# Expert layers fed by DMA regrouping and 32x32 VectorE transposes, with the first product two slots ahead

## The reference, cut to what matters

```
N, D, E, F = 3072, 384, 8, 1024            # tokens, model, experts, inner width
for e in range(E):
    for k in range(2):
        mask = top2[:, k] == e
        h = np.maximum(x[mask] @ w1[e], 0.0)
        out[mask] += top2_w[mask, k, None] * (h @ w2[e])
# then: rms norm, silu(xn @ w_gate) * (xn @ w_val) @ w_out, width 1536
```

## Time and profile before

| what | value |
|---|---|
| median of 3 runs | 1308.37 us |
| profiled execution, its own time | 1309.53 us |
| its span in the profile | 1307.8 us |
| TensorE busy | 1244.2 us (95%) |
| VectorE busy | 858.9 us (66%) |
| ScalarE busy | 458.4 us (35%) |
| GpSimd busy | 444.2 us (34%) |

### The profile page before, as it was taken

One profiled execution on the slowest core, in us unless ns is written; L12 is line 12 of the kernel. 1 busy time (PEld: TensorE's weight loads), 2 busy tenths in 40 slices (PEclk: granted clock), 3 DMA queues, 4 the chain that ended last, 5 costly groups with the idle time before them and its releaser, 6 DMA issues.

```text
span 1307.8 us, 26515 instructions
## 1 busy us (share of the span) xinstructions
PE 1244.2 (95%) x8915; PEld 1143.2 (87%) x8916; DVE 858.9 (66%) x1941; ACT 458.4 (35%) x982; POOL 444.2 (34%) x374
## 2 busy tenths in 40 slices
PE   4999999999899999999999998699999999999998
PEld 4777878777789989899998987599999999999997
DVE  7898888876578778787877876344454444444433
ACT  3565665654232222223222222233232323233221
POOL 8467777734641606061455530311010101010000
PEclk9999999999999999999999999699999999999999
DMA  5233433245413222232314310211010101010000
GB/s 214 87 97 127 131 124 119 65 165 224 145 50 133 84 99 99 85 113 73 132 48 161 140 43 25 73 37 37 19 55 1 55 19 37 19 36 18 0 19 19
DMA packets 36175, 105.46 MB, mean 81 GB/s; under 512 B 4992, under 2 KB 20352, under 8 KB 33664
## 3 DMA queue, kind: packets, MB, share of 16 engines
q1 hardware_dynamic: 27504, 56.41, 12.9%
q0 software_dynamic: 8592, 47.98, 10.3%
HBM read 77.83 MB, written 26.54 MB: 80 GB/s over the span
## 4 chain that ended last, share of the span: by engine, by line
PE 75%; DVE 7%; POOL 6%; issue 5%; ACT 5%; DMA 2%; another core or an unknown queue 0%; DVEq 0%; SPq 0%; ACTq 0%; POOLq 0%
PE pD L1776 12%; PE pD L1885 9%; PE pA L1885 9%; PE pA L1808 9%; PE pS L1808 8%; PE pA L1899 6%; PE pA L1584 5%; PE pA L1776 5%; PE pS L1899 3%; PE pA L1790 2%; PE pX L1749 1%; POOL qk L583 1%; DVE W L1087 1%; POOL prods L599 1%; DMA stage<-w 1%
## 5 line engine op out<-in xcount | busy, mean ns | idle before, releaser
L1520 DVE TENSOR_TENSOR gs<-pD,sig 128x384 f32<-128x384 f32 x96 | 53.5, 557 | 200.3 <-ACT sig L1022 200.3
L1263 DVE STREAM_TRANSPOSE pA<-pD 32x128 f32<-32x128 f32 x416 | 138.1, 332 | 54.6 <-PE pD L1776 48.9
L751 POOL DMA_INDIRECT pair<-y_sorted,y_row x48 | 46.5, 968 | 342.9 <-DVE z L1499 272.5
L1263 DVE STREAM_TRANSPOSE pA<-pA 32x128 f32<-32x128 f32 x400 | 132.8, 332 | 43.6 <-PE pA L1776 38.0
L926 ACT ACTIVATE hidH<-pA 128x512 fp32r<-128x512 f32 x110 | 65.8, 600 | 254.5 <-DVE pA L1263 244.9
L1584 PE MATMUL pA<-W 64*128 64x128 f32 (+3 forms) x1920 | 138.0, 284 | 16.3 <-DVE W L1087 13.0
L1776 PE MATMUL pD<-we,xsH 128*128 x462 | 145.6, 396 | 0.0
L1584 PEld LDWEIGHTS pA<-W 64*128 64x128 f32 (+3 forms) x1920 | 113.8, 171 | 35.5 <-DVE W L1087 18.7
L1022 ACT ACTIVATE sig<-pD 128x384 f32<-128x384 f32 x96 | 47.1, 491 | 211.2 <-PE pA L1885 211.1
L1808 PE MATMUL pA<-we,hidH 128*128 (+1 forms) x464 | 120.9, 342 | 0.0
L1087 DVE TENSOR_TENSOR W<-W,prods 128x512 f32<-128x512 f32 (+1 forms) x120 | 102.7, 862 | 20.9 <-PE pA L1584 17.1
(11 more groups left out here) (262 smaller groups left out, 2875.2 us busy)
## 6 DMA issues: line engine op xcount, KB each, us to landing
stage<-w POOLq DMA_DIRECT2D x14, 1536.0 KB
qk<-qk_t SPq DMA_DIRECT2D x24, 512.0 KB, 3.8
xs<-x_sorted SPq DMA_DIRECT2D x55, 192.0 KB, 2.4
y_sorted<-yo SPq DMA_DIRECT2D x55, 192.0 KB, 1.9
fT<-f_t SPq DMA_DIRECT2D x12, 512.0 KB, 5.7
vN<-v_n SPq DMA_DIRECT2D x24, 256.0 KB, 2.6
out<-fin SPq DMA_DIRECT2D x8, 576.0 KB, 2.8
stage<-w SPq DMA_DIRECT2D x2, 1536.0 KB
```

The source lines that it names most:

```text
L751: pool.indirect_dma_start(out=pair[:, j, k], out_offset=None, in_=y_sorted[:, :], in_offset=bass.IndirectOffsetOnAxis(ap=y_row[:, t * TS + ...
L1263: ins = dve.transpose(by_32[1][32 * q:32 * (q + 1), :, i], by_32[0][32 * i:32 * (i + 1), :, q])
L1520: dve.tensor_tensor(gs[:], pD[:, f % 2 * 512:f % 2 * 512 + TT], sig[f % 2][:], ALU.mult).then_inc(s_u, 1)
```

## The change

It does five things.

1. x, from slot 5 on: instead of one load of 128 rows, four loads (`in_quarters`). Load q fills partitions 32q to 32q+31: partition 32q+t gets, for each of four groups j, columns 96q to 96q+95 of row 32j+t. One VectorE instruction on 128x384 then turns all 32x32 blocks (`turn_x`), and the result in `pX` is the turned x, its columns taken with a step of 3; the rows of w1 are ordered to suit.
2. The middle activation, slots 5 to 53: relu of both halves, then a store of `hid` (128 x 4 KB) to `hid_rows` in device memory, then four loads by quarters back into `hidP`, then two VectorE instructions on 128x512 (`turn_hidden`). Slots 0 to 4 and 54 are turned by TensorE, eight transposes each.
3. TensorE's slot t is now `hidden(t+2)`, `output(t)`.
4. SyncE's slot t is now `load_hidden(t+1)`, `store_rows(t-1)`, `load_rows(t+4)`, `store_hidden(t+2)`.
5. GpSimd waits for the first product before it overwrites w1 and for the second before w2. In the last layer `combine` and the mean squares are spread, one group of 128 tokens for each of three steps f.

```diff
+def in_quarters(rows):
+    return rows.rearrange("(j t) (q c) -> q t j c", t=QP, q=Q)      # QP = 32, Q = 4
...
 # SyncE
             def load_rows(t):
                 row = sp.value_load(slot_i[0:1, 1, bass.ds(t.times(1), 1)], min_val=0, max_val=E * REGION - P)
-                sp.dma_start(xs[t.c % 4][:], x_sorted[bass.ds(row, P), :]).then_inc(s_xs[t.c % 4], 16)
+                of = x_sorted[bass.ds(row, P), :]
+                if x_by_pe(t): ...
+                for q in range(Q):
+                    sp.dma_start(xs[t.c % 4][QP * q:QP * (q + 1)].rearrange("p (j c) -> p j c", j=Q),
+                                 in_quarters(of)[q]).then_inc(s_xp[t.c % 4], 16)
+            def store_hidden(t):
+                wait_alone(sp, s_relu, t.times(2, 2))
+                if t.c >= FIRST_P + 2:
+                    wait_alone(sp, s_hp, (t - FIRST_P).times(16 * Q, -16 * Q))
+                sp.dma_start(hid_rows[t.par], hid[:]).then_inc(s_hs, 16)
+            def load_hidden(t):
+                wait_alone(sp, s_hs, (t - FIRST_P).times(16, 16))
+                wait_alone(sp, s_ht, t.times(1))
+                for q in range(Q):
+                    sp.dma_start(hidP[QP * q:QP * (q + 1)].rearrange("p (j c) -> p j c", j=Q),
+                                 in_quarters(hid_rows[t.par])[q]).then_inc(s_hp, 16)
             def slot(t):
-                if (t + 4).before(SLOTS):
-                    wait_alone(sp, s_tx, t.times(1, 1))
-                    load_rows(t + 4)
-                store_rows(t)
+                if (t + 1).before(SLOTS) and not hidden_by_pe(t + 1):
+                    load_hidden(t + 1)
+                store_rows(t - 1)
+                if (t + 4).before(SLOTS):
+                    wait_alone(sp, s_tx, t.times(1, 1))
+                    load_rows(t + 4)
+                if (t + 2).before(SLOTS) and not hidden_by_pe(t + 2):
+                    store_hidden(t + 2)
 # ScalarE, rectify: both halves, hid is free once its store has landed
+                elif t.c > FIRST_P:
+                    act.wait_ge(s_hs, (t - FIRST_P).times(16))
 # VectorE
+            def turn_x(t):
+                dve.wait_ge(s_xp[t.c % 4], (t - FIRST_P).over(4, 16 * Q, 16 * Q))
+                dve.wait_ge(s_xl, t.times(1))
+                dve.transpose(pX[:, 0:DM].rearrange("p (k j t) -> p k j t", k=KC, j=Q),
+                              xs[t.c % 4].rearrange("p (j f k) -> p k j f", j=Q, k=KC)).then_inc(s_tx, 1)
+            def turn_hidden(t, h):
+                if h == 0:
+                    dve.wait_ge(s_hp, (t - FIRST_P).times(16 * Q, 16 * Q))
+                dve.wait_ge(s_hl, t.times(2, h - 1))
+                k = FC // 2
+                dve.transpose(pA[0][:, h].rearrange("p (k j t) -> p k j t", k=k, j=Q),
+                              hidP.rearrange("p (j k f) -> p k j f", j=Q, k=FC)[:, h * k:(h + 1) * k]
+                              ).then_inc(s_ht if h else s_th, 1)
 # TensorE
             def slot(t):
-                if (t + 1).before(SLOTS):
-                    hidden(t + 1)
                 if (t + 2).before(SLOTS):
-                    turn_rows(t + 2)
-                if (t + 1).before(SLOTS):
+                    hidden(t + 2)
+                if (t + 1).before(SLOTS) and hidden_by_pe(t + 1):
                     turn_hidden(t + 1)
                 output(t)
```

More of the change, by code:

```diff
@@ L362, in program @@
         s_xs = [sem(f"s_xs{i}") for i in range(4)]
+        s_xp = [sem(f"s_xp{i}") for i in range(4)]
+        s_hs = sem("s_hs")
+        s_hp = sem("s_hp")
         s_ys = [sem(f"s_ys{i}") for i in range(2)]
@@ L420, in slots @@
         def slots(eng, body):
-            for n in range(EARLY, EARLY + 3):
+            for n in range(EARLY + 1, EARLY + 3):
                 body(Tile(n))
@@ L544, in _, with slot @@
             load_rows(Tile(4))
[L545 to L549, removed]
+            for n in (1, 2, 3):
+                wait_alone(sp, s_tx, n + 1)
+                load_rows(Tile(n + 4))
+                store_rows(Tile(n))
+            wait_alone(sp, s_tx, 5)
+            load_rows(Tile(8))
+            store_hidden(Tile(5))
+            load_hidden(Tile(5))
+            store_hidden(Tile(6))
+            def slot(t):
+                if (t + 1).before(SLOTS) and not hidden_by_pe(t + 1):
[6 more added lines that the diff above has]
+                    store_hidden(t + 2)
+            slots(sp, slot)
+            store_rows(Tile(SLOTS - 1))
             def store_tile(t):
@@ L974, in _ @@
             rectify(Tile(4))
+            high_x(Tile(6))
             for h in range(2):
                 high_h(Tile(4), h)
+            rectify(Tile(5))
+            high_x(Tile(7))
+            take_rows(Tile(4))
+            rectify(Tile(6))
+            for h in range(2):
+                high_h(Tile(5), h)
             def slot(t):
-                if (t + 1).before(SLOTS):
-                    rectify(t + 1)
+                if (t + 3).before(SLOTS):
+                    high_x(t + 3)
                 if (t + 2).before(SLOTS):
-                    high_x(t + 2)
+                    rectify(t + 2)
                 if (t + 1).before(SLOTS):
@@ L1038, in wide @@
                 for f in range(F2C):
-                    if f == 4 and (t + 1).before(NT2):
-                        mean_square(t + 1)
+                    if NEXT_SUM < f <= NEXT_SUM + TS and (t + 1).before(NT2):
+                        square_of(t + 1, f - NEXT_SUM - 1)
+                    if f == NEXT_SUM + TS + 1 and (t + 1).before(NT2):
+                        root(t + 1)
                     if NEXT_Z <= f < NEXT_Z + KC and (t + 1).before(NT2):
@@ L1454, in _ @@
             low_x(Tile(4))
+            turn_x(Tile(5))
             low_x(Tile(5))
[L1456 removed]
+            turn_x(Tile(6))
+            low_x(Tile(6))
             for h in range(2):
                 low_h(Tile(4), h)
+            turn_x(Tile(7))
+            low_x(Tile(7))
+            for h in range(2):
+                turn_hidden(Tile(5), h)
+            for h in range(2):
+                low_h(Tile(5), h)
             def slot(t):
+                if (t + 3).before(SLOTS):
+                    turn_x(t + 3)
+                    low_x(t + 3)
                 if (t + 1).before(SLOTS):
[L1462 to L1466 removed]
+                    if not hidden_by_pe(t + 1):
+                        for h in range(2):
+                            turn_hidden(t + 1, h)
                     for h in range(2):
@@ L1546, in wide @@
                 for f in range(F2C):
-                    if f == 3 and more:
-                        combine(t + 1)
-                    if f == 6 and more:
+                    if NEXT_SUM <= f < NEXT_SUM + TS and more:
+                        combine(t + 1, f - NEXT_SUM)
+                    if f == NEXT_Z - 1 and more:
                         norm(t + 1)
```

152 lines of the change are left out of this document (75 added, 77 removed).

## The result

The changed kernel takes 1318.77 us (median of 4 runs, 1315.43 to 1320.64), the kernel before, run beside it, 1308.51 us (4 runs, 1305.78 to 1309.28). The ratio is 1.0084, with a 95% interval of 1.0065 to 1.0102: slower by 0.8%, and the interval lies clear of the 0.3% bound. Forecast were 1322 us. The profiled execution took 1315.43 us, its span is 1314.0 us.

The account below looks back on a forecast made before the run. SyncE's queue was to bound the expert layer at 8.7 us a slot; with 43 us of delays the layer ends 18.0 later. 1309.5 + 18.0 - 4.0 = 1323.5 us profiled, given as 1322; range 1284 to 1375.

Parts of the forecast that it names:

- The bound moved to SyncE's queue: Expert layer: SyncE's ordered queue, ten DMAs a slot, sets the time at 8.7 us against TensorE's 8.38.
- The cycle, 8.7 us: SyncE's queue, one hidden store to the next: 2.6 + 1.9 + 0.7 + 2.9 + 0.5 + 0.1 us.
- The sign was forecast to turn at 8.4 us: SyncE's cycle in the expert layer: at 8.4 us, 47 cycles give 14 us and slower turns to faster.
- the queue keeps pace: Rival for the expert layer: cycle at most 8.38 us, TensorE sets it, only weight loads cost; 1299 us, chance 0.2.
- the lookahead's 6.9 us: Hidden's path through memory takes 9.9 of 16.8 us; the 6.9 us of slack is spent once.
- The delays, 43 us: Expert layer: hidden stores landing late beside weight loads, eight after the first, add 5 x 6.5 + 3 x 3.5 us.
- The five behind the experts' pairs: Hidden stores beside pairs of 1.5 MB weight loads: each landing put off by 6.5 us.
- The turn by packets: DMA queues taking turns per packet would make delays 15 us lower; rejected for the rows, rival at 1308, chance 0.1.
- The three behind the last layer's matrices: Hidden stores beside the 2.25 MB weight loads: each landing put off by some 3.5 us.
- The sum: Expert layer: first store at 363.5, cycles 408.9, delays 43, last slots; end at 832.4 us, 18.0 later.
- The last layer gave back: Last layer: spreading combine removes the eight waits behind it at f=3, 4.0 us less.
- the dear-quarters rival: SyncE's quarter loads cost up to 0.61 us each to issue, cycle 9.5 to 10.5; 1360 to 1407 us, chance 0.15.

Follow-up runs that it names:

- read_twice: The changed kernel with the row table read twice for each row load on SyncE's queue; 1353.23 us, ratio 1.0353 to the kernel before.
- rows_between: The changed kernel with SyncE's row loads, one slot further ahead, between hidden's store and its loads; 1277.40 us, ratio 0.9781 to the kernel before.
- small_weights: The changed kernel with the twelve weight loads for experts 2 to 7 moving only 16 columns each; 1282.31 us, ratio 0.9803 to the kernel before.
- the pieces experiment in after's order: The changed kernel, SyncE's order kept, with each weight load split by columns into four DMAs; 1312.95 us, ratio 1.0082 to the kernel before.
- x_only: The changed kernel with the middle activation turned by TensorE, only x through DMA quarters and VectorE; 1297.45 us, ratio 0.9954 to the kernel before.
- wide_only: The kernel before with only the last layer's combine and mean squares spread over three steps f; 1301.86 us, ratio 0.9956.

## Why the prediction was right, step by step

**The bound moved to SyncE's queue.** Right, and shown twice: 0.6 us more of register work made the cycle 0.6 us longer (read_twice), and the same ten DMAs a slot in another order gave back 41 us (rows_between). The first load comes 0.19 us behind the landing, as forecast, and the row loads stand directly before the store.

**The cycle, 8.7 us.** The mechanism right, the sum 0.35 us high: the undisturbed cycles are mostly 8.25 to 8.5, mean 8.35. The terms, forecast and measured: landing 2.6 and 2.64; wait before the loads 0.2 and 0.19; four loads 1.9 and 1.74; y store with its register work 0.7 and 0.63; y store's end to the row loads' end 2.9 and 2.76; wait before the store 0.3 and 0.30. These make 8.26, without the branch, which was put at 0.1. The landing was taken a little too low, the others at what they are or too high, the four loads and the row loads most (back to back the rows gave 0.49 us between starts, not 0.48). Over 47 cycles 16.4 us. The sign was forecast to turn at 8.4 us, and the cycle is below that: with 8.35 in it and all else as forecast, the sum gives a kernel 2 us faster than before. That it is slower nevertheless is due to the delays (7.3 us over the forecast) and the last slots (3.2 over), below. The first rival, "the queue keeps pace", had its condition met, a cycle of at most 8.38, and yet did not come true. Its first premise failed since TensorE's slot, too, is shorter than forecast (4.18 + 4.12 = 8.30), so that the queue stays just the longer of the two. Its second, that the lookahead's 6.9 us come off the delays, needs a queue that runs ahead; this one began at the landing of store(5) with nothing ahead and gained nothing on TensorE afterwards.

**The delays, 43 us.** Eight landings beside weight loads of 10.0, 7.9, 8.4, 9.6, 9.2, 8.0, 9.4 and 7.9 us made their cycles longer by 7.5, 5.8, 6.2, 6.9, 6.6, 5.2, 6.8 and 5.3 us: 50. The five behind the experts' pairs were forecast at 32.5 and measured 33.0; that this fits so well is partly luck, since the price came from a row load that meets the weight load in another way (see "The turn by packets"). The three behind the last layer's matrices were mis-sized: 17.3 us instead of 10.5. Their price had been read from a single row load and y store, issued at other moments of the load, and a store of 512 KB behind eight more DMAs does not meet it the same way. small_weights confirms the size of the five: 33.1 us less at the layer's end without them.

**The sum.** store_hidden(6) came at 363.1 (forecast 363.5), store_hidden(53) at 805.6 (815.4): 16.4 less from the cycle, 7.3 more from the delays, 0.4 from the start, which makes 9.5 of the 9.8. From there to the end of the layer took 20.2 us instead of 17.0, since TensorE, which last waited at 768.8 and then took 5.86 us for a product at the lower clock, was itself the later one from there on. The end, 825.8, is 6.6 under the forecast. The last layer gave back 4.9 instead of 4.0. So the forecast of 1322 us, 3 us from the 1318.8 measured, owes its closeness in part to errors that cancel: 16.4 us too much for the cycles against 7.3 and 3.2 too little for the delays and the last slots. The bound and the eight delays were right; that the sign came out right as well was a matter of a few us.

**The turn by packets.** Here the reason in the text was wrong, though the number it kept was right for the five pairs. The rows were said not to agree with the rule of the Trainium skill ("DMA: Bandwidth & Descriptors", Queues, rings and completion order), that each DMA engine takes turns between its queues packet by packet. They do take such turns. What the estimate of 3.4 us left out shows in before's queues between 453.4 and 456.7 us, where the weight load runs alone although a y store had been issued at 452.75 and a row load at 454.10:

```profile
q0 software_dynamic: 87, 1.07, 86.5%
```

Only from 456.8 us does the other queue appear beside it. So the y store waits 4 us, then has its eight packets per engine in turn with the weights' at 0.5 us each, nearly 4, and an end of 1.4 (the rest of the 1.9 us that it takes alone; an estimate): about 9, as in the earlier trace rows. The row load comes behind it in the same queue. In after the hidden store comes later in the load, and behind its own queue's backlog. The queues' tables of 582 to 589 us, beside the weight load, and of 590 to 594, when it is through, read

```profile
q0 software_dynamic: 218, 2.48, 92.2%
q1 hardware_dynamic: 219, 0.21, 9.7%
```

```profile
q1 hardware_dynamic: 1002, 1.03, 79.9%
q0 software_dynamic: 9, 0.00, 0.2%
```

219 packets against 218: turns one for one, so here the trace agrees with the rule. But in those 7 us the queue gets 14 packets per engine, and ahead of the store of 584.46 stand the pieces of three hidden loads (the first had landed at 581.2), a y store and four row loads: 24 + 8 + 32 per engine, less some six already served. So the store is served when the weight load is over, at about 590, and lands 4 us later. That also fits the pieces experiment in after's order: with packets of half the size the queue gets some more turns, but the load as a whole ends no sooner. The argument is from counts; no run changed the backlog alone. Nor does any run tell why the other queue is not served at the start of a load. In after it depends on the load: beside that of 512.92 the other queue gets next to nothing for 3.5 us, beside that of 578.90 it is served from the start.

**What needed no mending.** VectorE's transposes at 0.70 us (taken 0.75) lie in TensorE's shadow, with VectorE at 3.85 of 8.30 us. The quarters are issued in 0.32 to 0.43 us, no dearer than whole rows, so the dear-quarters rival fell with its first rows. GpSimd's edit costs nothing that a wait of TensorE's shows. TensorE's waits for ScalarE come with the late landings.

**What stays open.** The first product takes 4.12 or 4.13 us in the kernels built on after whose chain is shown here, also with transposes beside it (x_only), and 4.21 in before. That alone makes 4 us over the layer. In before the two halves are released by waits of their own and in after by others; none of the runs separates that.

## What to carry to other kernels

An engine that issues in order and must wait for the landing of its own store should have other issues to make in that time: the same ten DMAs cost 0.8% in one order and gained 2.2% in the other (the last layer's 0.4% is in both). A lookahead covers a delay only once; what counts is by how much the part that runs ahead (here the queue) is shorter than the one that sets the pace (here TensorE), since that alone refills it, and small delays beat one large only when it does. When work moves from a busy engine to DMAs, price the queue that issues them, instruction by instruction, and the landings beside the largest transfers of the kernel, before the engine's own saving.

## What the runs showed of the hardware that was not expected

- VectorE's transpose in 32x32 blocks takes 701 ns on 128x384 read with a stride and 705 ns on 128x512: the smaller one is no cheaper. On 32x128 it took 332 ns.
- A DMA by quarters with three dimensions on both sides costs SyncE 0.32 us (x) or 0.32 to 0.43 us (hidden) to issue, against 0.34 for a whole-row load.
- Beside each of the five pairs of weight loads in before, the y store issued 0.5 to 0.6 us ahead of the load's first packet and the row load behind it are not served for its first 3 to 3.5 us. In after this is so beside some loads and not beside others.
- Seven of TensorE's waits in after (1.9 to 6.6 us) are followed by a second product of 5.9 to 6.6 us instead of 4.18, with 0.50 granted right behind one of them (594.5 to 597.5 us). The layer ends 58 us later than the 767.9 that its products alone would give (771.7, less 0.08 for each of 48 first products): 41.9 are the waits, some 12 these seven products, and the rest is smaller.
- The length of the wait alone does not decide it. Before's last product of the layer came after a wait of 2.0 us and took 6.02 us, with 0.54 granted; that of wide_only came after the same wait, had 1.00 granted from 806 to 810 us, and took 4.52:

```profile
805.79 4.52 PE pS L1806 x24
```
